# Attention and two expert layers on one core: half of a weight matrix is rounded and split later, two scores and one load change places

## What is computed

```python
# attention: 2 x 8 heads, 768 positions, head size 64; 4 sink keys and a window of 128
keep = is_sink | in_window
scores = np.where(keep, scale * np.matmul(q, k.transpose(0, 1, 3, 2)), -1e9)
a = np.exp(scores - np.max(scores, axis=-1, keepdims=True))
attn_out = np.matmul(a / (np.sum(a, axis=-1, keepdims=True) + 1e-09), v)
x = attn_out.transpose(0, 2, 1, 3).reshape(B * S, H * D)      # 1536 x 512
h = x @ w_in                                                  # w_in 512 x 2048
x = (h - np.tanh(h)) @ w_out                                  # w_out 2048 x 512
# then a second layer of 8 experts (512 x 1024 x 512) of which each token takes its top 2
```

## Time and profile before

| | us |
|---|---|
| median of 3 runs | 709.51 |
| lowest, highest | 708.34, 709.69 |
| profiled execution, its own time | 710.72 |
| span of that execution in the trace | 709.0 |
| TensorE busy | 697.2 |
| GpSimd busy | 442.3 |
| VectorE busy | 361.3 |
| ScalarE busy | 218.7 |

### The profile page before, as it was taken

The page is one execution under the profiler, slowest core; times in us unless marked ns, Lnnn a source line. Parts: engine busy times, 40 slices in busy tenths (PEclk is TensorE's granted clock), DMA queues, the critical chain, the costliest instruction groups (busy, mean ns, idle before and its releaser), DMA issues.

```text
span 709.0 us, 12253 instructions
## 1 busy us (share of the span) xinstructions
PE 697.2 (98%) x3530; PEld 566.9 (80%) x3531; DVE 361.3 (51%) x821; ACT 218.7 (31%) x503; POOL 442.3 (62%) x272
## 2 busy tenths in 40 slices
PE   7999999999999999999999999999999999999997
PEld 5666788888888888888887888888888888888885
DVE  4788642222344222442266756556665565555654
ACT  7799632221422223322251212111211221122111
POOL 8899999000004000048569979969994999975472
PEclk9899999999999999999999999999999999999999
DMA  8743368000003000035183588687787987856677
GB/s 278 295 150 101 113 222 327 0 1 1 1 0 119 0 1 0 0 120 191 59 306 110 196 292 263 227 279 249 259 267 222 305 264 263 274 184 203 212 245 254
DMA packets 70257, 121.49 MB, mean 171 GB/s; under 512 B 8272, under 2 KB 36048, under 8 KB 69712
## 3 DMA queue, kind: packets, MB, share of 16 engines
q1 hardware_dynamic: 28272, 63.66, 26.8%
q10 hardware_dynamic: 38112, 44.84, 18.5%
q0 software_dynamic: 3840, 12.59, 5.5%
HBM read 81.74 MB, written 39.32 MB: 171 GB/s over the span
## 4 chain that ended last, share of the span: by engine, by line
PE 88%; POOL 4%; DVE 4%; another core or an unknown queue 1%; issue 1%; ACT 1%; DMA 0%; SPq 0%; DVEq 0%; POOLq 0%
PE bank L1784 23%; PE bank L1739 22%; PE bank L1597 18%; PE bank L1648 18%; POOL arena L735 2%; POOL arena L745 2%; DVE arena L1114 1%; PE bank L1543 1%; DVE arena L1136 1%; PE bank L1552 1%; PE bank L1751 1%; PE bank L1518 1%; PE bank L1670 1%; POOL arena L738 0%
## 5 line engine op out<-in xcount | busy, mean ns | idle before, releaser
L716 POOL TENSOR_TENSOR ring<-ring_raw,ring 128x2048 fp32r<-128x2048 f32 x32 | 147.7, 4615 | 2.5
L770 POOL DMA_INDIRECT sorted_x<-y_rows,arena x24 | 23.5, 978 | 184.2 <-DVE arena L1248 177.8
L1784 PE MATMUL bank<-ring,hidT_hi 128*128 (+1 forms) x448 | 138.3, 390 | 0.0
L714 POOL TENSOR_TENSOR ring<-ring_raw,ones 128x2048 fp32r<-128x2048 f32 x32 | 115.3, 3604 | 30.8 <-DMA ring_raw<-in_moe_w 30.7
L1739 PE MATMUL bank<-ring,xsT_hi 128*128 x464 | 124.3, 390 | 0.0
L1648 PE MATMUL bank<-gated_hi,w_out_sb 128*128 128x512 f32 x384 | 118.6, 390 | 0.0
L1739 PEld LDWEIGHTS bank<-ring,xsT_hi 128*128 128x128 f32 x464 | 87.0, 188 | 18.2 <-issue 0.3
L1182 DVE TENSOR_TENSOR bank<-bank,arena 128x512 f32<-128x512 f32 x48 | 33.6, 699 | 129.1 <-ACT arena L915 127.9
L1784 PEld LDWEIGHTS bank<-ring,hidT_hi 128*128 128x128 f32 x448 | 83.9, 188 | 17.3
L1784 PE MATMUL bank<-ring,hidT_lo 128*128 (+1 forms) x224 | 87.2, 389 | 0.0
L1648 PEld LDWEIGHTS bank<-gated_hi,w_out_sb 128*128 128x128 f32 x384 | 71.9, 188 | 14.8
(11 more groups left out here) (222 smaller groups left out, 1008.5 us busy)
## 6 DMA issues: line engine op xcount, KB each, us to landing
ring_raw<-in_moe_w SPq DMA_DIRECT2D x48, 512.0 KB, 5.3
hid_by_lane<-hid ACTq DMA_DIRECT2D x28, 512.0 KB
hid_lanes<-hid_by_lane ACTq DMA_DIRECT2D x28, 512.0 KB
ring_raw<-in_moe_w SPq DMA_DIRECT2D x8, 1024.0 KB, 6.9
sorted_y<-ys ACTq DMA_DIRECT2D x30, 256.0 KB
xs<-sorted_x ACTq DMA_DIRECT2D x100, 64.0 KB
sorted_y<-zeros SPq DMA_DIRECT2D x1, 4864.0 KB, 24.7
w_in_raw<-in_moe_w_in SPq DMA_DIRECT2D x2, 2048.0 KB, 10.3
```

What stands on the lines that cost most here:

```text
L714: pool.tensor_tensor(hi, raw, one_like(raw), ALU.mult).then_inc(rounded, 1)
L716: ins = pool.tensor_tensor(lo, raw, hi.bitcast(F32), ALU.subtract)
L770: pool.indirect_dma_start(out=sorted_x[:, :], out_offset=bass.IndirectOffsetOnAxis(ap=row_at[k][:, kk:kk + 1], axis=0), in_=y_rows_all[:, ...
L1784: last = pe.matmul(bank[into][:, :], x[:, c * P:(c + 1) * P], ring[:, bass.ds(at * 2 * WE + (w + CH * FE + c * DM), DM)], start=c == 0 and ...
```

## The change

Three things are done.

1. WIDE goes from 1024 to 512 columns, so w_in has 16 pieces, 0 to 7 in the first half and 8 to 15 in the second. During the attention, pass by pass, pieces 0 to 7 are rounded and split. ScalarE rounds pieces 8 to 15 in the dense layer, two behind each block_round(0, fc) for fc = 2 to 5, and GpSimd splits them one by one behind the w_out splits 2 to 9. hidden(0, 0) waits for 8 pieces in place of 4, hidden(0, 8) for 16 in place of 8.
2. In pass 1, scores 4 and 5 stand ahead of turn_probs(0, 1) on TensorE. VectorE's and ScalarE's copies of that turn move behind mask(1, 4) and exps(1, 4, 0).
3. ScalarE issues the load of pair 0's remaining queries behind its table load and warm-up.

```diff
-        WIDE = WE // PAIRS
+        WIDE = WE // (2 * PAIRS)
...
                     split(w_out_raw[:, fc, 1, :], w_out_sb[:, fc, 0, :], w_out_sb[:, fc, 1, :], splits, w_out_split)
+                    if 2 <= fc < 2 + PAIRS:
+                        split_w_in(PAIRS + fc - 2)
...
-            act.dma_start(qT[0][:, WIN:], q[0, :, WIN:]).then_inc(second_q, 16)
             act.wait_ge(pool_step, 1)
             act.activation(exp_warm[:, :], ones[:, 0:1], ACT.Exp)
+            act.dma_start(qT[0][:, WIN:], q[0, :, WIN:]).then_inc(second_q, 16)
...
                 exps(p, 3, 0)
-                if p >= 1:
+                if p >= 2:
                     probs_out(p - 1, 1)
...
                 if p >= 1:
-                    probs_out(p - 1, 2)
+                    probs_out(p - 1, 1 if p == 1 else 2)
                 exps(p, 4, 1)
                 exps(p, 5, 0)
+                if p == 1:
+                    probs_out(0, 2)
                 exps(p, 5, 1)
...
                 if fc < 2:
                     attn_out(PAIRS - 1, fc)
+                elif fc < 2 + PAIRS // 2:
+
+                    round_w_in(PAIRS + 2 * (fc - 2))
+                    round_w_in(PAIRS + 2 * (fc - 2) + 1)
...
                 inverse(p, 0)
-                if p >= 1:
+                if p >= 2:
                     probs_out(p - 1, 1)
-                if p >= 2:
                     attn_out(p - 2, 0)
                 mask(p, 4, 0)
                 mask(p, 4, 1)
+                if p == 1:
+                    probs_out(0, 1)
                 mask(p, 5, 0)
...
-                    pe.wait_ge(w_in_split, CH * (fc // HALF + 1))
+                    pe.wait_ge(w_in_split, PAIRS * (fc // HALF + 1))
...
                     second_end(p - 2)
-                if p >= 1:
                     turn_probs(p - 1, 1)
                 score(p, 4)
                 score(p, 5)
+                if p == 1:
+                    turn_probs(0, 1)
                 if p >= 1:
                     turn_probs(p - 1, 2)
```

## The result

Over five runs of each on the same chip the changed kernel takes 713.81 us (median; 713.12 to 715.17) and the kernel before 708.34 us (707.74 to 709.69). The ratio is 1.0068, with a 95% interval of 1.0050 to 1.0086: slower by 4.8 us, between 3.5 and 6.1, by this ratio; the two medians lie 5.5 us apart. The forecast was 713.6. The profiled execution took 713.55 us, with a span of 711.8; against the 709.0 of before that is only 2.8 more.

A forecast was written before the change was run, and what follows sets the result against it. TensorE, 98% busy, was taken as the bound, alone on the chain of waits from about 80.7 us. Terms -1.4 + 0 + 3.3 + 2.2 + 0 = +4.1 on a 709.5 median gave 713.6 us; 8-in-10 range 710.9 to 716.0.

The forecast's parts named there:

- The seam: From attention to dense layer: hidden(0, 0) waits for GpSimd's split of the eighth piece, starting at 86.2; +3.3 us.
- The clock at the seam: Behind TensorE's idle time at hidden(0, 0), the granted clock falls and work runs at half: +2.2 us, bounds 0 and 3.4.
- The second pair: Two scores fill TensorE's wait before turn_probs(0, 1); score(2, 0) starts near 21.15, set by its keys: -1.4 us.
- The later ask for the queries: At the start, loading pair 0's remaining queries near 2.3 us, landing between 5.5 and 7: 0, ends -0.3 and +0.6.
- The dense layer: First eight chunks: eight more GpSimd splits finish 0.7 us before hidden(0, 8); 0, bounds 0 and +0.8 us.
- The attention loop: Pairs 2 to 7: the shorter w_in split only lengthens GpSimd's idle time; period stays 9.51 us, 0 gained.
- rival D: Attention loop, pairs 2 to 7: GpSimd sets the pace, each period shrinks by 1.1 us, giving 706.9 us; chance 0.05.
- B: Rival at the seam from attention to dense layer: the clock holds, giving 711.4 us; chance 0.16.
- E: Rival: clock holds at the seam and pair 2's keys land earlier, score(2, 0) at 20; 709.9 us; chance 0.06.
- C: Rival: the start gives nothing, the clock falls before score(2, 0) and pair 2 runs low; 715.4 us; chance 0.13.

The follow-up runs named there:

- part 1 alone: The kernel before with only w_in's part of the change, start as before: 713.94 us, ratio 1.0058; run again in another group: 713.65 us, ratio 1.0076.
- both orders beside each other: The changed kernel and the kernel before with only w_in's part, run in one group: 713.80 us (ratio 1.0073) and 713.65 us (ratio 1.0076).
- The later rounding: The changed kernel with ScalarE's rounding of pieces 8 to 15 one chunk later: 720.38 us, ratio 1.0173.
- the finer waits: The changed kernel with hidden(0, 0) waiting for 7 pieces, hidden(0, 4) for 8, hidden(0, 8) for 15, hidden(0, 12) for 16: 709.14 us, ratio 0.9990.
- filler: The changed kernel with unread matmuls of ones in front of hidden(0, 0): six, 713.95 us, ratio 1.0054; twelve, 713.05 us, ratio 1.0041.
- the old order with the noise moved: The changed kernel with hidden(0, 0) waiting for 7 pieces, noise loads behind pair 4's, and the second pair's order of before: 708.56 us, ratio 0.9979.

## Why the prediction was right, and where it was not

**The seam, +3.3: right.** Idle time of 3.43 us in front of hidden(0, 0), released by the split of 1.26 us that was costed at 1.24. The mechanism is shown by making the count finer (ratio 0.9990) and by part 1 alone (1.0058).

**The clock at the seam, +2.2: right in kind, mis-sized; it measured 1.55.** The prediction took over the course of the earlier trace rows, a fall 0.9 us after the idle time began and 6.8 us at the low level. Here the clock fell 4.1 us after the idle time had begun (81.9 to 86.0), when TensorE was at work again, and was low for 3.4 us. All of it lay on work, a loss of 1.55 where half of 3.4 is 1.7. The failed step is the assumption that a second fall runs as the first; the bounds of 0 and 3.4 held it.

**The second pair, -1.4: too much; between 0 and -0.6 in the runs, which can't be told from nothing.** The step that failed is "22.88 - 21.15 = 1.7 us gained". It compared the new order with one execution of the old in which the clock was low; the old order without a fall stands at 21.14 and 20.86, where the prediction had 22.88. Nor does any run show the microsecond of low clock in pair 2 that was to take the 1.7 down to 1.4: with the new order and the noise loads in their old place, three profiled executions have 3.4 us of it there and five none. TensorE was also ready earlier than reckoned, at 19.59 (18.07 + 1.52) and not at 20 to 21.3. The keys' landing was named as the next limit, rightly, but it limits the old order too whenever the clock holds. With the noise loads in their old place the keys' landing itself moves by 2 us between executions, from 20.7 to 22.8, so that it isn't a fixed wall at 21.11. The issue moves by 1 us (16.07 to 17.09), and the time from there to score(2, 0) is 4.2 to 6.1. Of the -1.07 that the two profiled executions showed, nothing is left with both orders beside each other: it set one execution of before with a low clock against one of the changed kernel with late keys.

**The later ask for the queries, 0: right, by a wrong road.** ScalarE issued the load at 1.07 us, not at 2.3. The table load in front of it in the list didn't hold the issue up:

```profile
0.82 1.28 ACT L878 ACT_TABLE_LOAD   x1 [0.66 <-PEq L1873]
1.07 0.40 ACTq L879 DMA_DIRECT2D arena<-in_q  x1
```

It landed 2.7 us later, in time for pair 0's score 2.

**The dense layer, 0 with 0.7 to spare: right.** The last split ended at 129.35 and hidden(0, 8) started 0.55 us later, without a wait:

```profile
129.90 0.39 PE L1606 MATMUL bank<-xT_hi,w_in_hi 128*128 128x512 f32 x1
```

The later rounding shows that the room is not larger.

**The attention loop, 0: right.** The period stayed 9.51, and rival D is dead: the 1.1 us became idle time of GpSimd.

**Sum.** Forecast +4.1, TensorE's shift 3.98 in the profiled executions, 4.8 by the ratio with 3.5 to 6.1 as the interval, 5.5 between the medians. That 3.98 is near 4.1 is luck: it holds the -1.07 of the start, which the other runs don't bear out. The smaller loss at the clock and the missing gain at the start go opposite ways: with the sizes as measured the sum is 3.4 + 1.55 + 0 = 5.0, and the finer waits, which take the first two away, gave 4.8 to 5.5. That 713.6 came so near 713.8 is part luck: the kernel before ran at 708.34 beside the changed one and not at 709.51, and from there the forecast sum of 4.1 gives 712.4. Of the rivals, B (the clock holds at the seam) is refuted by every trace with the coarse wait and no filler; so is E, which needs B. C's low stretch in pair 2 came in three of eight profiled executions; it is no rarity, but not the usual course either. D is answered above.

## What to carry to other kernels

When a semaphore count stands for many small pieces, wait at each consumer for the pieces that it reads: here the change's whole loss was one count that took in a piece that the consumer did not need yet, and 7 in place of 8 gave back about 5 us. Read a possible gain from more than one execution, above all where the granted clock was low in the one at hand: a stall that only a low clock makes may not be there to be removed in other runs. When an engine waits for a transfer, look at what stands in front of it in the queue: moving three small tables with short rows gained 2.6 us, where reordering the work that waited gained nothing that the runs can tell.

## What the runs showed of the hardware

Up to 140 us every low stretch of TensorE's clock (0.50 granted) was 3.41 us long, but for the 6.8 us in the profiled execution of before (at the end of the span others stand that cost nothing: in the changed kernel the last matmul ends at 706.8 and the clock falls at 710.6). They begin during or behind idle times of 1.5 to 4.8 us, but not each such idle time has one. The 1.48 or 1.49 us at 14.5 was followed by a fall in two executions (before; the old order with the noise moved) and by none in two others (part 1 alone, both times). In front of score(2, 0), 2.01 us had one and 2.22 us had none. The 3.4 us at the seam had one in all seven traces in which nothing filled it, up to 1.5 us after work had begun again (84.62 to 86.08 in part 1 alone). At the seam a rest of 1.82 us behind 1.60 us of filler had one, 0.48 us behind 2.94 us had none.

The issue of a DMA on SyncE takes from 0.33 us to several, by where it stands: three noise loads take 4.94 us of issue at 10.5 and 1.53 us at 27.7, and with these moved away the load of pair 2's queries, 0.50 us in the changed kernel, took 2.90 at 10.17. What makes an issue long was not shown: the long ones stand where much is under way (the changed kernel moves 400 to 422 GB/s from 9 to 14 us), and no run took the large loads away. Nor do the runs separate the noise loads' issue from their transfers: in before the DMA share is 1.07 at 15.4 us with only 59 GB/s moved, in the changed kernel it is 0.68 with 37 GB/s.

The wait of 1.0 to 1.2 us for hidT_lo_last in the experts goes by the group: all traces of the two groups in which the kernel before had a median of 710.18 and 710.06 show it, none of the group at 708.53, nor that of the changed kernel beside 708.34. The same kernel differs by about 1.6 us from group to group, of which this wait would be the larger part; that is argued from single traces, and why it comes stays open. This is why ratios, and not times, are compared across groups.
